# Merging the own and the preceding block of keys in a sliding-window attention: scores, exponentials, turns and a value difference

## The reference, cut to what matters

```python
# q, k, v: (4, 8, 768, 64); n_sink = 4, window = 128
scores = scale * q @ k.T                        # scale = 1/8
keep = (pos_k < n_sink) | ((0 <= pos_q - pos_k) & (pos_q - pos_k < window))
scores = where(keep, scores, -1e9); scores -= max(scores)
a = exp(scores); a = a / (sum(a) + 1e-9); attn = a @ v
x = attn, the 8 heads beside each other         # (4, 768, 512)
theta = x @ w_theta; zr, zi = x*cos(theta), x*sin(theta)
u = x + w_tok_r @ zr + w_tok_i @ zi             # over the 768 tokens
x = u + relu(u @ w_ch)
gate = sigmoid(causal convolution of x, 5 taps); out = (gate * (x @ w_val)) @ w_out
```

## Time and profile before

| | |
|---|---|
| median of 3 runs | 658.61 us (657.82 to 658.89) |
| the profiled execution: its own time, span in the profile | 659.08 us, 657.4 us |
| PE, PEld | 642.3 us (98%), 549.4 us (84%) |
| DVE, ACT, POOL | 418.2 us (64%), 295.0 us (45%), 254.3 us (39%) |
| granted TensorE clock | 0.996 of full speed in the mean |

### The profile page before, as it was taken

The page is one execution under the profiler, slowest core; times in us unless marked ns, Lnnn a source line. Parts: engine busy times, 40 slices in busy tenths (PEclk is TensorE's granted clock), DMA queues, the critical chain, the costliest instruction groups (busy, mean ns, idle before and its releaser), DMA issues.

```text
span 657.4 us, 14120 instructions
## 1 busy us (share of the span) xinstructions
PE 642.3 (98%) x4016; PEld 549.4 (84%) x4016; DVE 418.2 (64%) x1008; ACT 295.0 (45%) x775; POOL 254.3 (39%) x323
## 2 busy tenths in 40 slices
PE   7999999999899999999999999999999999999995
PEld 5777777777688888888888888899999999999993
DVE  5887887878765365544646357869757457458450
ACT  6877877777443232232242323443344244243231
POOL 3745645645132212221131311356445445445420
PEclk9999999999899999999999999999999999999999
DMA  7667567566321136213522246330520220120011
GB/s 250 213 211 248 192 213 251 184 234 195 107 57 41 33 96 191 64 32 96 158 65 64 80 133 206 112 113 1 191 97 33 65 96 33 64 96 32 17 48 53
DMA packets 61337, 76.71 MB, mean 117 GB/s; under 512 B 4208, under 2 KB 41328, under 8 KB 61296
## 3 DMA queue, kind: packets, MB, share of 16 engines
q1 hardware_dynamic: 61296, 76.24, 35.9%
HBM read 51.06 MB, written 25.17 MB: 116 GB/s over the span
## 4 chain that ended last, share of the span: by engine, by line
PE 95%; issue 1%; DMA 1%; DVE 1%; POOL 0%; SPq 0%; POOLq 0%; ACT 0%; DVEq 0%
PE acc L1495 31%; PE ps_p L1544 18%; PE ps_th L1484 10%; PE ps_o L1584 10%; PE ps_s L501 8%; PE ps_t L527 7%; PE ps_y L550 7%; PE ps_o L564 2%; PE ps_x L1473 1%; PE ps_o L566 1%; DMA x_res<-xT_scratch 1%; DMA q_sb<-qT 1%; POOL g_lo L1146 0%; PE ps_t L510 0%; DVE k_big L1312 0%
## 5 line engine op out<-in xcount | busy, mean ns | idle before, releaser
L1114 POOL TENSOR_TENSOR z_lo<-z_raw,z_hi 128x512 fp32r<-128x512 f32 x48 | 63.2, 1338 | 206.7 <-ACT z_hi L1191 206.7
L1495 PE MATMUL acc<-w2h,z_hi 128*128 128x512 f32 (+1 forms) x384 | 131.2, 342 | 0.0
L1495 PE MATMUL acc<-w2l,z_hi 128*128 128x512 f32 (+1 forms) x384 | 129.3, 337 | 0.0
L1495 PE MATMUL acc<-w2h,z_lo 128*128 128x512 f32 (+1 forms) x384 | 129.3, 337 | 0.0
L333 ACT ACTIVATE probs<-masked,neg_max 128x260 f32<-128x260 f32 (+1 forms) x192 | 92.6, 484 | 33.9 <-DVE neg_max L400 33.8
L400 DVE CUSTOM_DVE_ANT_0 masked<-ps_s,mask 128x260 f32<-128x260 f32 (+1 forms) x192 | 68.9, 403 | 35.0 <-PE ps_s L501 31.0
L1495 PEld LDWEIGHTS acc<-w2h,z_lo 128*128 128x128 f32 x384 | 72.8, 190 | 8.0
L1495 PEld LDWEIGHTS acc<-w2l,z_hi 128*128 128x128 f32 x384 | 72.9, 190 | 7.8
L1495 PEld LDWEIGHTS acc<-w2h,z_hi 128*128 128x128 f32 x384 | 72.8, 190 | 7.8
L1305 DVE TENSOR_TENSOR xT_lo<-ps_x,xT_hi 128x512 fp32r<-128x512 f32 x24 | 16.6, 690 | 78.0 <-ACT xT_hi L1175 78.0
L1408 DVE SCALAR_TENSOR_TENSOR ps_g<-m_raw,conv_w,ps_g 128x384 f32<-128x384 f32 x112 | 62.0, 618 | 0.2
(11 more groups left out here) (93 smaller groups left out, 1456.4 us busy)
## 6 DMA issues: line engine op xcount, KB each, us to landing
v_sb<-vP SPq DMA_DIRECT2D x16, 384.0 KB, 4.5
x_scratch<-x_sb SPq DMA_DIRECT2D x16, 384.0 KB, 2.6
x_nat<-x_scratch SPq DMA_DIRECT2D x24, 256.0 KB, 2.8
xT_scratch<-xT_raw SPq DMA_DIRECT2D x24, 256.0 KB, 2.2
x_res<-xT_scratch SPq DMA_DIRECT2D x24, 256.0 KB, 3.2
uT_scratch<-u_sb SPq DMA_DIRECT2D x24, 256.0 KB, 2.6
uT<-uT_scratch SPq DMA_DIRECT2D x8, 768.0 KB, 4.6
out<-o_sb SPq DMA_DIRECT2D x24, 256.0 KB, 2.0
```

What stands on the lines that cost most here:

```text
L1114: nc.gpsimd.tensor_tensor(z_lo[s % ZR][:, part, :], z_raw[:, part, :], z_hi[s % ZR][:, part, :].bitcast(F32), ALU.subtract).then_inc(z_lo_ ...
L1495: last = nc.tensor.matmul(bank, l, r, start=first and s == 0 and m == 0 and a == 0, stop=s == T - 1 and m == 1 and a == 2, skip_group_chec ...
```

## The change

From the third tile on (visits B and C) the own block's scores are copied over the preceding block's where the own key is the one kept (`merge`, a predicated copy within PSUM). `mask_max`, the exponential and the turn then work on one block and the sinks: 132 columns for 260, 128 for 256. The transposes of B's and C's tiles fall from eight to four a turn. To multiply by the right values, the turned probabilities are kept twice: all of them, against the preceding block's values, and those of the own block (times a 0/1 mask `ownT`), against the difference own minus preceding, `v_over`, which GpSimd makes once per pair. `evac_y` of A and C moves from VectorE to ScalarE, and now stands between its second and third exponential. The scores themselves are made as before.

```diff
-            ps_s = [[ps(f"ps_s{e}{t}", [P, 512]) for t in range(2)] for e in range(2)]
+            ps_s = [ps(f"ps_s{t}", [P, 2, 512]) for t in range(2)]
+        def both_heads(m):
+            return ps_t[m - 1][:].rearrange("p t (h q) -> p (t h) q", q=P).rearrange("p (e t) q -> p e t q", e=2)
@@ gpsimd @@
+            def values_over(n, s, it):
+                pool.wait_ge(v_in[s], 16 * (it + 1))
+                wait_count(pool, pv_done, VISITS * (n - 1))
+                pool.sem_inc(pool_gate, 1)
+                nc.gpsimd.tensor_tensor(v_over[s][:], v_sb[s][:, 2:T, :], v_sb[s][:, 1:T - 1, :],
+                                        ALU.subtract).then_inc(v_over_done, 1)
             def step(it, first=False):
...
+                    values_over(n, s, it)
                     split_sinks(n, s, it)
@@ scalar @@
-                lo, hi = columns(i)
+                lo, hi = columns(i) if v == 0 else (0, OWN)
...
+                    act.wait_ge(evac_v, k + 1)
+                    nc.scalar.copy(probsT[:, :, 2 * m:2 * m + 2, 0:P], both_heads(m)).then_inc(evac_a, 1)
...
-                        for t in range(2):
-                            for e in range(2):
-                                exp(n, s, v, t, e)
-                        if v == 1 and not (first and s == 0):
-                            evac_y(n - 1)
+                        for e in range(2):
+                            exp(n, s, v, 0, e)
+                        if not (first and s == 0):
+                            evac_y(n - 1, v)
+                        for e in range(2):
+                            exp(n, s, v, 1, e)
@@ vector @@
-                dve.wait_ge(scores, g + 1)
+                if v > 0:
+                    lo, hi = 0, OWN
+                    dve.wait_ge(merged, 4 * n + 2 * v + t - 1)
+                else:
+                    dve.wait_ge(scores, g + 1)
+            def merge(n, v, t):
+                dve.wait_ge(scores, SCORES * n + 4 * v + 2 * t + 2)
+                dve.sem_inc(dve_gate, 1)
+                nc.vector.copy_predicated(ps_s[t][:, :, 0:P],
+                                          early.own[:].bitcast(U32).unsqueeze(1).to_broadcast([P, 2, P]),
+                                          ps_s[t][:, :, OWN:KEYS]).then_inc(merged, 1)
             def evac(k, m):
-                dve.wait_ge(turned, 2 * k + 1)
+                dve.wait_ge(turned, 2 * k + (2 if m > 0 else 1))
                 if m > 0:
-                    nc.vector.tensor_copy(probsT[0][:, 2 * m:2 * m + 2, :], ps_t[0][:]).then_inc(evac_v, 1)
+                    nc.vector.tensor_tensor(probsT[:, :, 2 * m:2 * m + 2, P:2 * P], both_heads(m),
+                                            early.ownT[:].unsqueeze(1).unsqueeze(1).to_broadcast([P, 2, 2, P]),
+                                            ALU.mult).then_inc(evac_v, 1)
...
+                        if v > 0:
+                            merge(n, v, 0)
+                            merge(n, v, 1)
                         for t in range(2):
                             for e in range(2):
                                 mask_max(n, s, v, t, e)
...
-                        if v != 1 and started:
-                            evac_y(n - 1, v)
@@ tensor @@
                     for t in range(2):
                         i = 2 * m + t
+                        if m > 0:
+                            last = nc.tensor.transpose(both_heads(m)[:, e, t, :], probs[e][:, i, 0:P], ident[:])
+                            continue
...
-                passes = [(2 * m, at + P, 0, 2 * P), (2 * m + 1, at + 3 * P, P, P)]
-                if m > 0:
-                    passes.append((2 * m - 1, at, 0, P))
+                if m == 0:
+                    passes = [(v_sb[s][:, 0], 0, P, 2 * P, 0), (v_sb[s][:, 1], 1, P, P, P)]
+                else:
+                    pe.wait_ge(v_over_done, n + 1)
+                    passes = [p for t, i in enumerate((2 * m, 2 * m + 1))
+                              for p in ((v_sb[s][:, i - 1], i, 0, P, t * P), (v_over[s][:, i - 2], i, P, P, t * P))]
@@ Early.gpsimd @@
-        for m in (self.mask0, self.mask1, self.mask):
+        for m in (self.mask0, self.mask1, self.none):
             pool.memset(m[:], 0.0).then_inc(self.zeroed, 1)
+        for m in (self.own, self.ownT):
+            pool.memset(m[:], 1.0).then_inc(self.zeroed, 1)
```

More of the change, by code:

```diff
@@ L127, in fast_path @@
         probs1, at = row("probs1", [P, T, W], F32, at)
-        probsT0, at = row("probsT0", [P, T, 2 * P], F32, at)
-        probsT1, at = row("probsT1", [P, T, 2 * P], F32, at)
-        probs, probsT = [probs0, probs1], [probsT0, probsT1]
+        probsT, at = row("probsT", [P, 2, T, 2 * P], F32, at)
+        probs = [probs0, probs1]
         sink_probs, at = row("sink_probs", [P, P], F32R, at)
@@ L155, in fast_path @@
         w_raw = x_nat[2:6]
-        mask, mask1, mask0 = early.mask, early.mask1, early.mask0
+        mask1, mask0 = early.mask1, early.mask0
+        v_over = [place(nc, f"v_over{s}", [P, T - 2, P], F32, Z_AT + 4 * (T - 2) * P * s) for s in range(2)]
         with ExitStack() as banks:
@@ L176, in fast_path @@
         scores = sem("scores")
+        merged = sem("merged")
         maxed = sem("maxed")
@@ L351, in evac_sinks, with evac_y @@
                 nc.scalar.copy(sinkT[:], ps_t[1][:, 0, 0:P]).then_inc(sink_evac, 1)
[L353 to L357, removed]
+            def evac_y(n, m):
+                act.wait_ge(pv_done, VISITS * n + m + 1)
+                wait_count(act, y_turned, VISITS * (n - 1) + m + 1)
+                nc.scalar.copy(y_sb[m][:], ps_y[:, 0:2 * P]).then_inc(y_evac[m], 1)
             def step(it, first=False):
@@ L378, in _ @@
             mix.xT(0, 0)
+            evac_y(PAIRS - 1, 0)
             evac(VISITS * PAIRS - 1, VISITS - 1)
-            evac_y(PAIRS - 1)
+            evac_y(PAIRS - 1, 1)
             evac_sinks(PAIRS - 1)
             mix.xT(0, 1)
+            evac_y(PAIRS - 1, 2)
             mix.sines(0, 0)
@@ L462, in _ @@
             mix.begin()
-            evac_y(PAIRS - 1, 0)
             mix.xT(0, 0)
@@ L500, in qk @@
                         wait_count(pe, maxed, g - 3)
-                        nc.tensor.matmul(ps_s[e][t][:, lo:hi], q_sb[s][rows, i * P:(i + 1) * P],
+                        nc.tensor.matmul(ps_s[t][:, e, lo:hi], q_sb[s][rows, i * P:(i + 1) * P],
                                          k_sb[s][rows, first:first + hi - lo], start=True, stop=True
                                          ).then_inc(scores, 1)
-            def free_turn_bank(e, k):
-                wait_count(pe, (evac_v, evac_a)[e], k)
             def turn_sink(n):
@@ L541, in pv @@
                 pe.wait_ge(evac_a, k + 1)
-                at = 2 * m * 2 * P
-                passes = [(2 * m, at + P, 0, 2 * P), (2 * m + 1, at + 3 * P, P, P)]
-                if m > 0:
-                    passes.append((2 * m - 1, at, 0, P))
-                for a, (j, src, dst, width) in enumerate(passes):
+                if m == 0:
+                    passes = [(v_sb[s][:, 0], 0, P, 2 * P, 0), (v_sb[s][:, 1], 1, P, P, P)]
[3 more added lines that the diff above has]
+                              for p in ((v_sb[s][:, i - 1], i, 0, P, t * P), (v_over[s][:, i - 2], i, P, P, t * P))]
+                for a, (values, i, at, width, dst) in enumerate(passes):
                     for e in range(2):
                         rows = slice(D * e, D * (e + 1))
-                        keysT = probsT[e][:].rearrange("p t k -> p (t k)")[:, src:src + width]
-                        last = nc.tensor.matmul(ps_y[rows, dst:dst + width], v_sb[s][:, j, rows], keysT,
+                        src = 2 * P * i + at
+                        keysT = probsT[:, e].rearrange("p t k -> p (t k)")[:, src:src + width]
+                        last = nc.tensor.matmul(ps_y[rows, dst:dst + width], values[:, rows], keysT,
                                                 start=a == 0, stop=a == len(passes) - 1, skip_group_check=True)
@@ L683, in _ @@
             sp.dma_start(words[:], limits.bitcast(I32).to_broadcast([P, 4])).then_inc(limits_in, 16)
-            for first in (early.q_in, early.k_in, early.v_in):
+            for first in (early.q_first, early.k_first, early.q_in, early.k_in, early.v_in):
                 sp.wait_ge(first, 16)
@@ L1671, in __init__ @@
         self.mask1 = place(nc, "mask1", [P, KEYS], F32, at + 512)
-        self.mask = place(nc, "mask", [P, KEYS], F32, at + 512 + 1056)
-        self.q_first, self.k_first, self.q_in, self.k_in, self.v_in, self.zeroed, self.masks_step, self.masks_done, self.ident_done = (
+        self.none = place(nc, "none", [P, P + FAST_SINK], F32, at + 512 + KEYS_PITCH)
+        self.own = place(nc, "own", [P, P], F32, at + 512 + KEYS_PITCH + 544)
+        self.ownT = place(nc, "ownT", [P, P], F32, at + 512 + KEYS_PITCH + 544 + 512)
+        (self.q_first, self.k_first, self.q_in, self.k_in, self.v_in, self.zeroed, self.masks_step, self.masks_done,
```

(1 more changed line is left out.)

45 lines of the change are left out of this document (23 added, 22 removed).

## The result

The changed kernel takes 666.71 us in the median of 4 runs (664.70 to 667.92), the kernel before 658.75 (657.82 to 659.02). The ratio is 1.0117, 95% interval 1.0102 to 1.0131: 8 us slower. The forecast was slower, 661.4, range 653 to 671: the direction and the mechanism came out, the size is nearly three times what I said. Run again beside later experiments, the changed kernel took 666.40 and the kernel before 659.23, ratio 1.0111 (1.0084 to 1.0138).

A forecast was written before the change was run, and what follows sets the result against it. The prediction took the TensorE-VectorE ring to bound B and C after the change, matmuls A: 0.30 us more a pair, +4.2 over 14 pairs, -1.4 once, on 659.08 gives 661.9, so 661.4 for the median; range 653 to 671.

The forecast's parts named there:

- the ring in visit C: Chain through TensorE and VectorE: scores, merge, four `mask_max`, `normalise`, `turn_y`, next scores; 3.75 us in C, against 3.49 before.
- the four `mask_max`: On VectorE in B and C, narrowed to 132 columns: 0.27 us each, 1.08 for four, against 1.40 before.
- the way from `turn_y` back to the next scores: TensorE's last part of the ring: 0.36 us in B, 0.46 in C.
- the -1.4 for what comes once: Outside the looped pairs: fewer transposes and an unqueued last `evac_y` save, start memsets cost; sum -1.4 us.
- What bounds: Before: matmuls bound A, the ring B, and C has 0.28 us of slack; after, the ring lengthens B and C.
- The rival that matmuls still bound everything: All removed transposes gained, 14 us, giving 644.6 us; chance 0.05.
- Transposes: TensorE, visits A and C: four fewer save 0.44 us, A falling to 2.67; in C only the ring decides; B gains nothing.
- The merge: VectorE, B and C: 0.39 us per 256-column merge; the second starts 1.35 after the visit begins, hiding the first.
- The slow-merge rival: A merge takes two cycles a column or more, B and C 0.5 us longer, 671 us; chance 0.14.
- The visits: Visit lengths after the change: A 2.67, B 3.92, C 3.75 us; a pair 10.34, against 10.04 before.
- The sum: +4.2 us over 14 looped pairs, -1.4 once, on 659.08: 661.9 profiled, 661.4 for the median.
- ScalarE, GpSimd, the clock in the attention: Forecast not to bound; ScalarE or TensorE's clock as rivals gave about 675 us, joint chance 0.08; GpSimd's added 1.3 us hidden.

The follow-up runs named there:

- e1: The changed kernel with `normalise` moved ahead of the merges in visits B and C: 644.75 us, 0.9793 of the kernel before.
- e2: The kernel before with the same move of `normalise` alone, ahead of `mask_max`: 655.40 us, 0.9952 of the kernel before.
- e3: The changed kernel with VectorE's loop written out, so its counts are constants: 660.78 us, 1.0038 of the kernel before.
- e7: The changed kernel with TensorE's loop written out and VectorE's kept: 664.85 us, 1.0085 of the kernel before.
- e11: The changed kernel run once more, unaltered, beside e9 and e10: 666.40 us.
- e9: The changed kernel with the output copies of visits A and C back on VectorE, behind `normalise`: 666.82 us.
- e10: As e3, and the 1e-9 not added to the row sums, so that instruction is left out: 659.63 us, 1.0011 of the kernel before.
- e4: The changed kernel without GpSimd's difference `v_over`, multiplying by the own block's values instead: 665.73 us.
- e6: The changed kernel with `normalise` moved as in e1 and VectorE's loop written out as in e3: 644.24 us, 0.9769 of the kernel before.
- e5: The changed kernel without the merges, the own block's scores left out from the third tile on: 652.18 us, 0.9889 of the kernel before.

## Why the prediction was right, and where its size was wrong

The step that failed is a sum: the ring in visit C, 1.35 + 0.39 + 1.08 + 0.42 + 0.05 + 0.46 = 3.75. Two of its terms were too small, the four `mask_max` (1.08) and the way from `turn_y` back to the next scores (0.46), and C came out at 3.91 and 4.03. A second term, the -1.4 for what comes once, shows in the profiled executions and hardly in the medians. The parts of the ring, medians over the looped pairs (us):

| part | forecast B, C | even B | odd B | even C | odd C |
|---|---|---|---|---|---|
| visit's start to the first `mask_max` | 1.74, 1.74 | 1.67 | 1.67 | 1.68 | 1.69 |
| first `mask_max` to `normalise` | 1.08, 1.08 | 1.20 | 1.08 | 1.24 | 1.18 |
| `normalise` to `turn_y` | 0.74, 0.47 | 0.75 | 0.75 | 0.48 | 0.48 |
| `turn_y` to the next scores | 0.36, 0.46 | 0.36 | 0.36 | 0.52 | 0.69 |

- **What bounds.** Right. The ring bounds B and C after the change, matmuls A; e1 shows it by opening the ring. The rival that matmuls still bound everything is out: C's transposes were gained in e1 only.
- **Transposes.** Right: A fell by 0.44 (3.06 to 2.62), C by 0.43 once the ring was open (e1 against e2).
- **The merge.** Right: next start 0.34 after it, where I took 0.39; its record is 0.43 against 0.48. The second one starts 1.34 after the visit began, where I took 1.35. The slow-merge rival is out.
- **mask_max.** Too small. I took 0.27 each, 1.08; it took 1.20 and 1.08 in B, 1.24 and 1.18 in C. e3 shows that what exceeds 0.88 is nearly all the counts. I had seen that C needs two more of them and then took one number for B and C. Over the 14 pairs the term is 2.7 us short, and the quicker merges give 1.8 back. The page of the Trainium skill that I drew on, "VectorE: DVE Perf Modes", its section on the TRN2 errata, led me to estimates of 262 ns for a narrow `mask_max` and 392 for a merge. With constant counts (e3) the next instruction starts 0.21 to 0.24 after a narrow `mask_max`, and 0.34 after a merge, both less than that; their records, 0.29 and 0.43, are longer than that. For a ring the starts count, and the measurements decide.
- **From the wait back to work.** Too small. In C `turn_y` to the next scores takes 115.61 - 115.10 = 0.51, not the 0.46 it took with no wait before it, and 0.68 in odd pairs, by TensorE's loop jump (e7). That is 2.0 us over the 14 pairs.
- **The visits.** C is 3.91 and 4.03 where I said 3.75: (0.16 + 0.28) x 7 = 3.1 us of the error. B came out at 3.92 in the mean, as said, in part by luck: its `mask_max` took 0.06 more than I counted and its merges 0.07 less.
- **Held-up row sums.** Not in the sum of the forecast. They stand right ahead of C's merges. In one C of the changed kernel:
```profile
100.40 1.27 POOL L290 TENSOR_TENSOR v_split<-v_sink,v_split 64x512 fp32r<-64x512 f32 x1 [0.18 <-POOL v_split L286]
...
100.74 0.96 DVE L453 TENSOR_SCALAR row_sum_g<-row_sum 128x12 f32<-128x12 f32 x1
101.74 0.23 DVE L455 RECIPROCAL inv_sum<-row_sum_g 128x12 f32<-128x12 f32 x1
101.95 0.76 DVE L434 COPY_PREDICATED ps_s<-own,ps_s 128x256 f32<-128x256 uint32 x2
```
A sum over 12 columns takes 0.96 us and ends at 101.70, as GpSimd's product ends (101.67); undisturbed it takes 0.16 (at 111.66). That C lasted 4.21. `mask_max` is not held: its 0.30 stays 0.30 while the same GpSimd product runs (109.65 to 110.92). The mean over odd C is 0.04 above its median: 0.3 us in all. In the kernel before the same happened (up to 0.90), nearly all under cover of VectorE's idle time: the C with the 0.90 took 3.55 in place of 3.49. The Trainium skill ("GPSIMD Engine Reference", section "Specifications") says that GpSimd shares its SBUF interfaces with VectorE and contends with VectorE instructions that run in a two-port mode or have two SBUF inputs; the row agrees that there is contention, and none here shows which mode the sum ran in.
- **Once only.** I took -1.4. The loop gives (10.59 - 10.03) x 14 = 7.8 us, and the two profiled executions' own times differ by 5.6 (664.70 and 659.08), so -2.2 remains there: -0.8 before the loop, -0.3 between it and the next stage, and -1.1 behind, 0.7 of it with the spell of half clock that the changed kernel's execution lacks. In the medians, which are 8.0 apart, little of the -1.4 is left. The changed kernel's profiled executions here (664.70, and 665.42 in e11) are the shortest of their four and both lack the spell; e7, e9 and e10 have it. The other runs have no profile, but each has its mean granted clock on record: of the changed kernel's eight, five have 0.998 and a median of 665.87 us, three have 0.994 or 0.996 and 667.56; of the 28 of the kernel before beside the experiments, 16 have 0.997 or more and 658.5 us, 12 have less and 659.6. That fits the spell, so it may be a part of the 2 us by which the median lies over the first profile; it is not shown.
- **The sum.** 661.4 and 5.3 short: 3.5 in the loop (0.3 of it the row sums), 1.6 in what comes once, and 0.2 in the base.
- **ScalarE, GpSimd, the clock in the attention.** None bounds; with waits of 0.4 to 0.8 us in each B and C the granted clock stayed at full speed (1.00 from 31 to 155 us; a spell at 0.50 comes only in the last 3 us of the execution, when TensorE has no more work). e4 and e9 agree for the other two engines.

## What to carry to other kernels

Look in the sums of waits for a small wait that comes in every turn: it marks the ring that closes next, and the work that an edit removes from another engine is then waited away. Before shortening the instructions of such a ring, ask whether a member of it can be done in the idle time ahead: here moving `normalise` ahead of the scores' wait was worth 3 us in the kernel before and 22 in the changed one, and only with it is the merging a gain (644.75 us, 2.1% under the kernel before; constant counts, e6 at 644.24, add nothing that can be told). In this kernel's hardware loop a short instruction followed its predecessor by what the sequencer needs for its counts, not by its columns: 132 columns took 0.33 us with one count and 0.22 with constants.

## What the runs showed that I had not expected

- 132 columns of `mask_max` in the loop cost 0.33 us each with one count (e5), 0.22 to 0.39 with shared ones, 0.21 to 0.24 with constants (e3); 260 columns cost 0.35.
- A wait just ahead of a loop's jump costs more than its length: 0.68 in place of 0.52 us to the next matmul (the changed kernel and e7), and nothing where there is no wait (e1). The kernel before lost its 0.11 of every second A when the wait in B went (e2), though a whole visit C lies between that wait and the jump; why is not shown.
- A 0.16 us instruction on VectorE, the row sums' addition, takes up to 1.16 us (e3) and 1.22 (e5) while a long GpSimd one runs, and ends 0.03 to 0.04 after it.
